# A linear-attention and two-layer expert kernel: the norm's inverse root and weights moved from the tokens to the gates, the probabilities and the up weights

## The reference

```python
# 1: attention with decay, B=2, H=8, S=768, D=64
state = gamma * state + outer(k[t], v[t]);  y[t] = scale * (q[t] @ state)
# x = y of all heads side by side: 1536 tokens x 512
# 2: norm, then a gated layer with 1536 hidden columns
rms = np.sqrt(np.mean(x * x, axis=-1, keepdims=True) + 1e-06)
xn = x / rms * rms_g
g = xn @ w_gate
x = (g * sigmoid(g)) * (xn @ w_val) @ w_out
# 3: four experts of 1024 hidden columns, mixed by probabilities
p = domain_probs / (domain_probs.sum(-1, keepdims=True) + 1e-09)
out = sum over e of p[:, e] * (np.maximum(x @ w1[e], 0) @ w2[e])
```

## Time and profile before

| | |
|---|---|
| median of 3 runs | 853.41 us (852.61 to 854.93) |
| profiled execution | 852.45 us |
| its span, first to last instruction | 850.7 us |
| mean granted TensorE clock | 0.997 of full speed |
| busy: PE, DVE, ACT, POOL | 834.2, 477.0, 236.4, 403.0 us |
| first matmul of unit 0 / of unit 3 | 54.11 / 90.14 us |

### The profile page before, as it was taken

The page is one execution under the profiler, slowest core; times in us unless marked ns, Lnnn a source line. Parts: engine busy times, 40 slices in busy tenths (PEclk is TensorE's granted clock), DMA queues, the critical chain, the costliest instruction groups (busy, mean ns, idle before and its releaser), DMA issues.

```text
span 850.7 us, 12760 instructions
## 1 busy us (share of the span) xinstructions
PE 834.2 (98%) x4840; PEld 772.4 (91%) x4840; DVE 477.0 (56%) x777; ACT 236.4 (28%) x463; POOL 403.0 (47%) x440
## 2 busy tenths in 40 slices
PE   9997999999999999999999999999999999999998
PEld 8777999999999998888989989899899889898897
DVE  4598544555555458775554554554554545545545
ACT  1565322222233225322221222222222222212221
POOL 3797753637271838733836236336336326325100
PEclk9999999999999999999999999999999999999999
DMA  9821010001010010100201101101100100110003
GB/s 349 294 107 50 25 51 26 25 32 44 25 50 26 25 50 25 50 1 21 78 2 49 50 1 50 50 1 50 50 13 37 50 34 18 50 50 1 26 11 137
DMA packets 13451, 44.45 MB, mean 52 GB/s; under 512 B 1488, under 2 KB 1616, under 8 KB 13392
## 3 DMA queue, kind: packets, MB, share of 16 engines
q1 hardware_dynamic: 13104, 43.00, 14.2%
q10 hardware_dynamic: 288, 0.64, 0.2%
HBM read 40.49 MB, written 3.15 MB: 51 GB/s over the span
## 4 chain that ended last, share of the span: by engine, by line
PE 59%; DVE 1%; issue 0%; ACT 0%; DVEq 0%
PE bank L508 20%; PE bank L507 20%; PE bank L506 19%; DVE x_sum L230 0%; DVE x_lo L234 0%; DVE h_lo L952 0%; ACT x_hi L687 0%; DVE x_all L978 0%; DVE out_acc L993 0%; DVE out_acc L989 0%; DVE c L919 0%; DVE bank L912 0%; ACT u L692 0%; DVEq L977 0%; DVEq L911 0%
## 5 line engine op out<-in xcount | busy, mean ns | idle before, releaser
L506 PE MATMUL bank<-x_hi,w_hi 128*128 128x384 f32 x784 | 264.3, 337 | 9.0 <-DVE x_lo L234 4.8
L508 PE MATMUL bank<-x_lo,w_hi 128*128 128x384 f32 x784 | 263.6, 336 | 0.0
L507 PE MATMUL bank<-x_hi,w_lo 128*128 128x384 f32 x784 | 263.5, 336 | 0.0
L993 DVE SCALAR_TENSOR_TENSOR out_acc<-bank,p_norm,out_acc 128x512 f32<-128x512 f32 x180 | 134.9, 749 | 127.7 <-PE bank L508 127.7
L506 PEld LDWEIGHTS bank<-x_hi,w_hi 128*128 128x128 f32 x784 | 147.8, 188 | 17.1 <-issue 9.6
L507 PEld LDWEIGHTS bank<-x_hi,w_lo 128*128 128x128 f32 x784 | 147.6, 188 | 5.4
L508 PE MATMUL bank<-wd_lo,h_hi 128*128 128x512 f32 x384 | 151.6, 395 | 0.0
L507 PE MATMUL bank<-wd_hi,h_lo 128*128 128x512 f32 x384 | 151.2, 394 | 0.0
L506 PE MATMUL bank<-wd_hi,h_hi 128*128 128x512 f32 x384 | 149.5, 389 | 1.0 <-DVE out_acc L989 1.0
L508 PEld LDWEIGHTS bank<-x_lo,w_hi 128*128 128x128 f32 x784 | 147.6, 188 | 0.0
L336 POOL TENSOR_TENSOR w_lo<-w_raw,w_hi 128x256 fp32r<-128x256 f32 x196 | 141.3, 758 | 3.1 <-ACT w_hi L659 0.9
(11 more groups left out here) (69 smaller groups left out, 868.9 us busy)
## 6 DMA issues: line engine op xcount, KB each, us to landing
w_raw<-wu SPq DMA_DIRECT2D x28, 512.0 KB, 4.4
ring<-qkv SPq DMA_DIRECT2D x23, 512.0 KB, 7.6
wd_raw<-wd SPq DMA_DIRECT2D x22, 512.0 KB, 3.5
out<-out_acc SPq DMA_DIRECT2D x12, 256.0 KB, 2.0
y_decay<-t_y_decay SPq DMA_DIRECT2D x6, 256.0 KB, 4.9
ring<-qkv ACTq DMA_DIRECT2D x1, 512.0 KB, 7.6
small_sb<-small ACTq DMA_DIRECT2D x1, 114.0 KB, 5.1
```

Of the source, the lines that this page charges most:

```text
L506: pe.matmul(dst, s_hi, m_hi, start=first, stop=False, skip_group_check=True)
L507: pe.matmul(dst, s_lo, m_hi, start=False, stop=False, skip_group_check=True)
L508: return pe.matmul(dst, s_hi, m_lo, start=False, stop=last, skip_group_check=True)
L993: nc.vector.scalar_tensor_tensor(out=to, in0=new, scalar=p, in1=to, op0=ALU.mult, op1=ALU.add).then_inc(posted, 1)
```

## The change

The tokens are no longer multiplied by anything before the first layer:

- The inverse root is kept in a tensor of its own, `rstd` (negative, by the form of the refinement), one value for each token on all partitions. A new `scale_gate` on VectorE multiplies the gate sums by it before the silu, twice in each of the 24 units. The value half keeps its missing factor through the layer; it passes the relu unchanged, as it is positive, and is put back in the second layer's probabilities: `turn_rstd` on TensorE turns the row of 1536 values into columns by 12 matmuls of one column in unit 2, and `scale_probabilities` multiplies `p_norm` by them, once.
- The norm's weights become a factor of the up weights' rows: `scale_w` on ScalarE, four instructions for each of the 12 pairs c of the first layer, in `w_raw`, before GpSimd's sums.
- `normalise` is gone (16 instructions on VectorE), and so is one ScalarE instruction of each guess.
- What waited for the normalised tokens now waits for `y_taken`. Parts and sums of the tokens stand earlier and in another order; the remainders of A11 (both halves) and of A22 (first half) move from GpSimd to VectorE. The load of pair 1 stands one step earlier in SyncE's queue, before the keys of step 11. `w_raw` has seven blocks instead of eight. GpSimd's remainders of tokens are done in two instructions each. `hidden` and its splits run in the order a = 0, 1 instead of 1, 0.

```diff
-WS = {"T1": 0, "T2": 1, "T3": 2, "T4": 3, "B11": 4, "B21": 5, "B22": 6, "B12": 7}
+WS = {"T1": 0, "T2": 1, "T4": 2, "B11": 3, "B21": 4, "B22": 5, "T3": 6, "B12": 6}
...
-                elif n == 11:
+                elif n == 10:
                     load_w(1)
...
             def sum_w(c):
-                pool.wait_ge(w_in, 16 * (c + 1))
+                if c < F1:
+                    pool.wait_ge(w_scaled, KT * (c + 1))
+                else:
+                    pool.wait_ge(w_in, 16 * (c + 1))
                 w_op("T1", "B12", "B11")
+                pool.wait_ge(w_sums, 4 * c + 1)
                 w_op("T3", "B22", "B12")
-                pool.wait_ge(w_sums, 4 * c + 1)
                 w_op("T2", "B22", "T1")
...
-                operand_lo(nc.gpsimd, k, name).then_inc(x_ready[name], 1)
+                if k == 1 and name[0] == "A":
+                    pool.wait_ge(y_done, NSTEP)
+                operand_lo(nc.gpsimd, k, name, slice(0, 1))
+                operand_lo(nc.gpsimd, k, name, slice(1, 2)).then_inc(x_ready[name], 1)
...
-                    part_lo(0, "A11")
+                    split_w_lo(0, 4, NP)
...
-                    split_w_lo(0, 4, NP)
+                    part_lo(0, "A12")
...
-                    part_lo(0, "A12")
+                    sum_w(1)
...
-                    part_lo(0, "A22")
+                    split_wd_lo(0)
...
-                    sum_w(1)
-            split_wd_lo(0)
-            split_w_lo(1)
-            part_lo(1, "A11")
+                    split_w_lo(1, 0, 4)
+            split_w_lo(1, 4, NP)
...
+            def turn_rstd():
+
+                pe.wait_ge(rstd_step, 4 * J)
+                for n in range(NSTEP):
+                    mm = pe.matmul(bank[7][:, n:n + 1], rstd[0:1, n // SPB, CH * (n % SPB):CH * (n % SPB) + CH],
+                                   ones[0:1, 0:1], start=True, stop=True)
+                mm.then_inc(rstd_turned, 1)
...
                 if name == "M1" and 2 <= q < Q1 + 2:
-                    pe.wait_ge(h_ready, 2 * (q - 2) + 1)
+                    pe.wait_ge(h_ready, 2 * (q - 2) + 2)
...
                 elif name == "M5" and 2 <= q < Q1 + 2:
-                    pe.wait_ge(h_ready, 2 * (q - 2) + 2)
+                    pe.wait_ge(h_ready, 2 * (q - 2) + 1)
...
-                pe.wait_ge(h_ready, h_count(max(units)) + 2 - a)
+                pe.wait_ge(h_ready, h_count(max(units)) + 1 + a)
                 if n == 0:
-                    pe.wait_ge(x_normal, 16)
-                elif n >= 2:
+                    pe.wait_ge(rstd_step, 4 * J)
+                elif n == 1:
...
                 if q == 0:
                     sum_squares(3)
+                product(q, f, j, k, "M6")
+                if q == 2:
+                    turn_rstd()
                 product(q, f, j, k, "M2")
...
+            def scale_w(c):
+
+                act.wait_ge(w_in, 16 * (c + 1))
+                for kt in range(2):
+                    for half, blocks in enumerate((slice(WS["B11"], WS["B12"] + 1, WS["B12"] - WS["B11"]),
+                                                   slice(WS["B21"], WS["B22"] + 1))):
+                        r = 2 * half + kt
+                        nc.scalar.activation(w_raw[:, blocks, kt, :], w_raw[:, blocks, kt, :], ACT.Copy,
+                                             scale=g_sb[:, r:r + 1]).then_inc(w_scaled, 1)
...
                 act.wait_ge(norm_done, k + 1)
-                sums = norm_bank(k)
-                nc.scalar.activation(guess[:, k % 2, :], sums, ACT.Ln, scale=1.0 / DM, bias=eps[:, :]).then_inc(guess_ready, 1)
-                nc.scalar.activation(sums, sums, ACT.Identity, scale=1.0 / DM, bias=eps[:, :]).then_inc(mean_ready, 1)
-
...
+                                     bias=eps[:, :]).then_inc(guess_ready, 1)
                 act.wait_ge(guess_ready, 3 * k + 1)
...
                 elif k < 2:
-                    act.wait_ge(x_normal, 8 * k + (8 if name == "A22" else 4))
-                    if k == 1:
-                        act.wait_ge(y_done, NSTEP)
+                    act.wait_ge(y_taken, SPJ * k + (SPJ if name == "A22" else SPB))
+                    if k == 1 and name != "A22":
...
-                if a == 0:
-                    act.wait_ge(c11_ready, q + 1)
-                    nc.scalar.activation(gate[:, s, :], bank[3 * s + 2][:, 0:TB], ACT.Silu).then_inc(silu_ready, 1)
-                else:
-                    act.wait_ge(up_done, up_count(q, "M4"))
-                    nc.scalar.activation(bank[3 * s][:, 0:TB], bank[3 * s][:, 0:TB], ACT.Silu).then_inc(silu_ready, 1)
+                act.wait_ge(gate_scaled, 2 * q + a + 1)
+                src = bank[3 * s + (0 if a else 2)][:, 0:TB]
+                nc.scalar.activation(src if a else gate[:, s, :], src, ACT.Silu, scale=-1.0).then_inc(silu_ready, 1)
...
                 copy_up(q, "M6", u2)
+                if q % 4 == 0:
+                    scale_w(q // 2 + 1)
                 silu(q, 0)
                 copy_up(q, "M7", u3)
+                if q % 4 == 1 and q // 2 + 2 < F1:
+                    scale_w(q // 2 + 2)
                 silu(q, 1)
+                copy_up(q + 1, "M1", m1)
+                hidden_hi(q, 0)
                 hidden_hi(q, 1)
-                if q + 1 < Q1:
-                    copy_up(q + 1, "M1", m1)
-                hidden_hi(q, 0)
...
-                if n == 4:
+                if n == 3:
+                    scale_w(0)
+                    part_hi(0, "A11")
+                elif n == 4:
+                    guess_rstd(0)
+                elif n == 5:
                     split_w_hi(0)
-                elif n == 5:
...
-                    part_hi(0, "A22")
+                    scale_w(1)
...
                 dve.wait_ge(guess_ready, 3 * k + 3)
-                nc.vector.scalar_tensor_tensor(out=mean, in0=guess_sq[:, k % 2, :], scalar=-0.5, in1=mean,
-                                               op0=ALU.mult, op1=ALU.mult).then_inc(rstd_step, 1)
+                nc.vector.scalar_tensor_tensor(out=sums, in0=sums, scalar=DM * EPS_RMS, in1=guess_sq[:, k % 2, :],
+                                               op0=ALU.add, op1=ALU.mult).then_inc(rstd_step, 1)
                 dve.wait_ge(rstd_step, 2 * k + 1)
-                nc.vector.scalar_tensor_tensor(out=mean, in0=mean, scalar=1.5, in1=guess[:, k % 2, :],
-                                               op0=ALU.add, op1=ALU.mult).then_inc(rstd_step, 1)
-
-            def normalise(k, first=0, last=KT):
-                j, a = k // 2, k % 2
+                nc.vector.scalar_tensor_tensor(out=rstd[:, k, :], in0=sums, scalar=1.5, in1=guess[:, k % 2, :],
+                                               op0=ALU.subtract, op1=ALU.mult).then_inc(rstd_step, 1)
+
+            def scale_gate(q, a):
+
+                k = 2 * UNITS1[q][1] + a
                 dve.wait_ge(rstd_step, 2 * k + 2)
-                for r in range(first, last):
-                    nc.vector.scalar_tensor_tensor(out=x_all[j][:, r, a, :], in0=x_all[j][:, r, a, :],
-                                                   scalar=g_sb[:, r:r + 1], in1=norm_bank(k),
-                                                   op0=ALU.mult, op1=ALU.mult).then_inc(x_normal, 1)
+                if a:
+                    dve.wait_ge(up_done, up_count(q, "M4"))
+                else:
+                    dve.wait_ge(c11_ready, q + 1)
+                src = bank[3 * (q % 2) + (0 if a else 2)][:, 0:TB]
+                nc.vector.tensor_tensor(src, src, rstd[:, k, :], ALU.mult).then_inc(gate_scaled, 1)
+
+            def scale_probabilities():
+
+                dve.wait_ge(rstd_turned, 1)
+                dve.wait_ge(setup, 5 + NE)
+                nc.vector.scalar_tensor_tensor(out=p_norm[:, :, :], in0=p_norm[:, :, :], scalar=-1.0,
+                                               in1=bank[7][:, 0:NSTEP].unsqueeze(1).to_broadcast([P, NE, NSTEP]),
+                                               op0=ALU.mult, op1=ALU.mult).then_inc(setup, 1)
...
             def hidden_all(q):
-                hidden(q, 1)
+                scale_gate(q, 1)
                 c12(q)
                 hidden(q, 0)
+                hidden(q, 1)
+                hidden_lo(q, 0)
                 hidden_lo(q, 1)
-                hidden_lo(q, 0)
...
                 c11(q)
+                scale_gate(q, 0)
...
             unit1(3, (0, 0, sum(EARLY)), LATE)
             end = F1 // 2 - 1
```

187 lines of the change are left out of this document (98 added, 89 removed).

## The result

The changed kernel takes 868.07 us (867.42 to 869.02, 4 runs) against 853.01 us (852.23 to 854.93, 4 runs): 1.0171 times the kernel before, 95% interval 1.0151 to 1.0191. Slower, as forecast; the forecast of 863.5 was 4.6 us too low. The profiled execution has a span of 867.0 us at a mean granted clock of 0.990 (before: 850.7 and 0.997), so 16.3 us have to be found in it.

A forecast was written before the change was run, and what follows sets the result against it. TensorE, busy 98% of the span, was taken as the bound, losing time only by waits, own work or clock. Terms summed to +10.1 on 852.45, 862.5; the median 0.96 above gave 863.5 us, range 853.5 to 870.5.

The forecast's parts named there:

- F: Change of layers: two scale_gate ahead of the remainders that unit 24 waits for, +1.1 us (0.5 to 2).
- A: Second sum of squares: TensorE waits for GpSimd's add behind pair 0's later high parts, +3.7 us (3.2 to 4.5).
- B: Third sum of squares: pair 1's scaling and weight sums stand ahead of GpSimd's add, +2.3 us (1.2 to 3.5).
- C: Units 0 to 2: waits for normalised tokens go, four new waits on ScalarE remain, -4.6 us (-9.8 to 0).
- D: Unit 2: the turning's 12 one-column matmuls, 24 instructions in TensorE's own stream, +1.7 us (0.8 to 4.5).
- E: Units 5, 9, 13, 17, 21: weight remainders late because sums wait for scale_w, +4.3 us (0 to 6.5).
- G: TensorE's clock: one fall again, as costly as before, after waits close together, +1.6 us (0 to 4).
- rival "no change": Whole kernel: the front costs what units 0 to 2 win, E hidden, no clock fall, 852 us; chance 0.11.
- more of the same: Units 0 to 2: backlogs give nothing back and the clock falls twice more, 868 to 872 us; chance 0.14.

The follow-up runs named there:

- kernel of A, B and E together: Changed kernel with split_w_hi(0) and scale_w placed earlier, split_w_hi(1) and sum_w(1) later; 853.76 us, 1.0001 times the kernel before.
- experiment on E: Changed kernel with scale_w ahead of the copy of M6 in the first unit of each weight pair; 862.11 us, 1.0098 times the kernel before.
- the short gate: Against the changed kernel with early scale_w (862.11 us), unit 23's two scale_gate multiply 8 columns instead of 384; 862.39 us.

## Why the prediction was right, and where its sizes were off

The sign and its main reason held: the added work of ScalarE and GpSimd stands ahead of what TensorE waits for. That the total came as near as it did is in part luck, since the wrong sign of F (2.2 us) hid part of what the clock cost: without it the time would have been some 870.3, at the very end of the range. The term by term account, in us:

| term | forecast | measured | |
|---|---|---|---|
| A | 3.7 | 4.1 | held: high parts 32.62, remainders 34.38 as forecast; the add's end 40.25 instead of 39.5, for which 0.3 was allowed |
| B | 2.3 | 3.4 | mis-sized |
| a late load of keys | 0 | 0.8 | a term that was missing |
| C | -4.6 | -5.2 | held: 4.6 of 9.8 are left, not 5.2; four waits of 0.2 to 1.24 at the four places named |
| D | 1.7 | 2.8 | mis-sized |
| E | 4.3 | 4.5 | held: five waits at the units named |
| F | 1.1 | -1.1 | wrong sign |
| G, clock | 1.6 | 7.4 | mis-sized |

Before rounding they add up to 16.5, against 16.3 on the spans (the tail gives back 0.2). Three sums of the forecast are off by a little and change nothing: B's 54.0 less 52.2 is 1.8, not 1.9; the first copy of M7 in C comes to 1.3, not 1.2; and the rival "no change" took B at 1.9 where its own term is 2.3, so it would give 852.4.

**B.** Two steps were too small. One was "take and square 1.5": TensorE's outputs were there at 50.0, and VectorE's take came 1.2 later, behind the sum and the remainder. I had counted what the change takes from VectorE and not looked at where in its queue the new work stands. The other was the price of GpSimd's work beside VectorE: the sums took 3.67 and the add 1.44 instead of 2.95 and 0.7, together 1.5 more. (The outputs were 2.9 us after the 47.1 of the forecast, by A and the slow clock behind it, but that moves TensorE and what it waits for alike.) The price of four `scale_w`, 1.7, was measured as 1.69. That A and B are two causes and not one was shown by undoing each.

**The keys.** The load of pair 1 waits until pair 0 is split, and it now stands ahead of the keys of step 11 in SyncE's queue: it was issued at 47.55 and the keys at 48.03, and TensorE waited 0.78 us for them. With the splits early again, in the kernel of A, B and E together, no such wait is left there.

**D.** The price of a one-column pair came from the nearest cheap row, 0.07 us an instruction; it is 0.12. The 24 take 2.83 us in each of the five other executions that have them in one row; in the changed kernel's the clock fell while they ran (granted 0.71 from 93 to 94), which makes them 3.16. The row of the experiment on E (TensorE):

```profile
91.36 2.83 PE L504 MATMUL bank<-ones,rstd 1*128 1x1 f32 x24
```

By the rule of the Trainium skill (TensorE: Matmul & The Clock Gate, LDWEIGHTS) that the prediction cites, the term would have been 2.6, an estimate, which is nearer.

**E.** Held in place and size; the experiment shows that it is the place in ScalarE's queue alone, since moving only that took all five waits away.

**F.** The failing step was to price only what was added in front of unit 24. The two `scale_gate` cost nothing there (the short gate: no change), and unit 24's wait for S3 was 0.72, not near 2.8. The halving of GpSimd's remainders, which stands in the diff and which the forecast does not mention, gains 1.1 in the changed kernel and 2.3 in the kernel before. How much the order of the work adds is open: the stretch takes 62.9 to 63.0 us in four profiled kernels of the changed order and 63.7 to 63.9 in six, by the wait of 0.73 to 0.76 that comes in some and not in others.

**G.** This is the largest miss: one fall as costly as before was forecast, and three came, two at the waits A and B, together 4.2, and one at the turning, 3.1. That the clock falls twice more was my rival "more of the same" (868 to 872, chance 0.14), and the time lies in its range. The falls are no fixed price: see below.

What is left open: why the clock falls in one execution and not in the next, and whether the turning itself brings its fall about; what the halves do to VectorE that whole instructions do not; and how much of their 2.9 us in units 0 to 3 is clock.

## What to carry to other kernels

Where a change adds work to engines that have slack on average, draw up the queue of each at the points where the bounding engine waits on it, and put the new work behind the last thing that is waited for; here that order was worth 14.3 us, and with it mended the change came out even with the kernel before. Mend chained queues together, since one moved alone moved the wait. And read the whole diff for instruction lengths too: an instruction cut in half on GpSimd sped up its neighbour VectorE.
